# Transposes of the mixture tile loop and of the last stage moved from TensorE to VectorE's 32x32 blocks

## What is computed

```python
x = attention(q, k, v)                    # (1536, 512)
e_idx, gate_w = argmax and softmax weight of x @ w_gate + bias
for e in range(8):                        # one expert per token
    h = np.maximum(x[mask] @ w1[e], 0.0)  # 512 -> 1024
    out[mask] = gate_w[mask, None] * (h @ w2[e])
h = np.maximum(out @ w_in, 0.0)           # 512 -> 2048
return h * h @ w_out                      # 2048 -> 512
```

## Time and profile before

| | before |
|---|---|
| median of three runs | 523.38 us |
| profiled execution, its own time | 523.15 us |
| its span (first to last instruction) | 521.5 us |
| TensorE busy | 510.0 us, 98% |
| VectorE busy | 225.3 us, 43% |
| ScalarE busy | 187.6 us, 36% |
| GpSimd busy | 87.3 us, 17% |
| mean granted TensorE clock | 0.995 |

### The profile page before, as it was taken

How to read it: one execution, slowest core, us unless ns; L and a number is a source line. 1 busy time by engine, 2 the same in 40 slices (tenths; PEclk the granted TensorE clock), 3 DMA queues, 4 the chain that set the end, 5 groups by cost and what they waited for, 6 DMA issues and landing times.

```text
span 521.5 us, 9415 instructions
## 1 busy us (share of the span) xinstructions
PE 510.0 (98%) x3115; PEld 411.3 (79%) x3117; DVE 225.3 (43%) x440; ACT 187.6 (36%) x355; POOL 87.3 (17%) x110
## 2 busy tenths in 40 slices
PE   8899999999999999999999999999999999999995
PEld 3587888878888888888788888888888888888884
DVE  3795786975323544237542422442242234222221
ACT  1875675235423555225522212331221233122121
POOL 4433336017600132200000000300000020000002
PEclk9998999999999999999999999999999999999999
DMA  8999757275571555520200000400000020000002
GB/s 280 308 267 336 258 196 260 79 291 137 124 281 40 201 206 216 192 91 29 94 1 1 0 1 0 161 0 0 0 0 0 0 80 0 0 0 0 0 0 80
DMA packets 19018, 54.92 MB, mean 105 GB/s; under 512 B 2848, under 2 KB 3120, under 8 KB 18480
## 3 DMA queue, kind: packets, MB, share of 16 engines
q1 hardware_dynamic: 11200, 27.47, 16.9%
q0 software_dynamic: 5200, 23.62, 12.4%
q10 hardware_dynamic: 2592, 3.49, 1.8%
HBM read 42.51 MB, written 12.07 MB: 105 GB/s over the span
## 4 chain that ended last, share of the span: by engine, by line
PE 91%; DMA 5%; DVE 2%; ACT 1%; issue 1%; POOLq 0%; POOL 0%; ACTq 0%
PE psum L1652 9%; PE psum L1653 9%; PE psum L1651 9%; PE psum L1667 8%; PE psum L1668 8%; PE psum L1669 8%; PE psum L1535 5%; PE psum L1560 5%; PE psum L1558 5%; PE psum L1537 5%; PE psum L1559 5%; PE psum L1536 5%; DMA q_in<-in_q 3%; PE psum L1568 2%; PE psum L1455 2%; PE psum L1370 2%
## 5 line engine op out<-in xcount | busy, mean ns | idle before, releaser
L1325 DVE TENSOR_TENSOR sq<-r_sb 128x512 f32<-128x512 f32 x48 | 33.2, 692 | 141.5 <-ACT r_sb L733 137.4
L733 ACT ACTIVATE r_sb<-psum 128x512 f32<-128x512 f32 x48 | 28.7, 597 | 143.8 <-PE psum L1653 143.8
L1667 PE MATMUL psum<-W,s_hi 128*128 128x512 f32 x192 | 75.9, 395 | 0.1
L1652 PE MATMUL psum<-z_lo,W 128*128 128x512 f32 x192 | 75.8, 395 | 0.0
L1653 PE MATMUL psum<-z_hi,W 128*128 128x512 f32 x192 | 75.8, 395 | 0.0
L1651 PE MATMUL psum<-z_hi,W 128*128 128x512 f32 x192 | 75.7, 394 | 0.0
L1668 PE MATMUL psum<-W,s_hi 128*128 128x512 f32 x192 | 75.5, 393 | 0.0
L1669 PE MATMUL psum<-W,s_lo 128*128 128x512 f32 x192 | 75.4, 393 | 0.0
L892 POOL DMA_INDIRECT out<-o_sb,sorted_m x12 | 11.6, 967 | 293.3 <-DVE o_sb L1341 291.4
L1327 DVE TENSOR_TENSOR s_lo<-sq,s_hi 128x512 fp32r<-128x512 f32 x48 | 33.2, 692 | 33.5 <-ACT s_hi L735 33.5
L735 ACT ACTIVATE s_hi<-sq 128x512 fp32r<-128x512 f32 x48 | 30.3, 632 | 41.8 <-DVE sq L1325 41.8
(11 more groups left out here) (205 smaller groups left out, 733.0 us busy)
## 6 DMA issues: line engine op xcount, KB each, us to landing
raw<-in_w POOLq DMA_DIRECT2D x4, 2048.0 KB, 9.8
raw<-in_w_io POOLq DMA_DIRECT2D x4, 2048.0 KB, 8.0
v_in<-in_v SPq DMA_DIRECT2D x12, 390.0 KB, 13.3
raw<-in_w SPq DMA_DIRECT2D x8, 512.0 KB, 5.4
kT<-in_kT SPq DMA_DIRECT2D x8, 400.0 KB, 8.0
q_in<-in_q SPq DMA_DIRECT2D x12, 256.0 KB, 9.1
X<-in_vT SPq DMA_DIRECT2D x4, 768.0 KB, 12.3
x_in<-xs_d SPq DMA_DIRECT2D x12, 256.0 KB, 2.7
```

The lines of the kernel that those rows point to most:

```text
L1325: dve.tensor_tensor(sq[:, :], r_sb[:, :], r_sb[:, :], ALU.mult).then_inc(sem["sqs"], 1)
L1652: pe.matmul(bank[f % 2][:, :], wh, z_lo[:, k, :], start=False, stop=False)
L1667: pe.matmul(bank[2 + j][:, :], s_hi[f % SBUFS][:, tok], wh, start=(f == 0), stop=False)
```

## The change

Twelve transposes of TensorE in each step of the tile loop, the 16 of the first group and the 32 of the other two go away. In their place:
- **x.** The load of a tile's rows (from tile 4 on) lands by quarters: partition q*32 + a holds four rows' quarter q of the columns. VectorE then transposes all 32x32 blocks with one instruction (`x_turn`) into `x_w`, which is the memory of `x_lo`; reads and writes step four elements. ScalarE and VectorE split it there.
- **h.** After each half's relu, SP spreads it with four DMAs from `h_sb` to `h_q` (SBUF to SBUF, `spread_h`), and VectorE transposes it (`h_turn`) into `h_w`, the memory of `h_lo`. The first half waits until the first half of `layer2(t - 1)` is done, the second half for its end.
- **z.** The rows of each group land by quarters with four DMAs; VectorE transposes with four instructions a group. The gate is not multiplied on the way in; its square is multiplied onto the output instead (the copies at the end of a group take a scale).
- **Order.** On VectorE, the copy of y comes after both halves of `h_lo`; y has two PSUM banks (4 and 7), and the last `layer2` follows `layer2(n_t - 2)` directly. The rows of w1, w2 and w_in are put in the order 4p + k on the host. TensorE's remaining transposes (tiles 0 to 3) read their operand with a step of four elements.

```diff
             def load_x(t, s):
-                sp.dma_start(x_in[s][:, :], xs_d[bass.ds(row, P), :]).then_inc(s_xs[s], 16)
+                    sp.dma_start(x_in[s][:, :], xs_d[bass.ds(row, P), :].rearrange("(a j) (q f) -> q a j f", a=QW, f=P)
+                                 ).then_inc(s_xs[s], 16)
+            def spread_h(t):
+                for h in range(2):
+                    sp.wait_ge(sem["relu"], t * 2 + (h + 1))
+                    for q in range(KD):
+                        sp.dma_start(h_q[h][q * QW:(q + 1) * QW, :], quarter(h_sb[:, h * DM:(h + 1) * DM], q)
+                                     ).then_inc(s_hq[h], 16)
+            def load_z(g, into):
+                for q in range(KD):
+                    sp.dma_start(into[q * QW:(q + 1) * QW, :], quarter(ys_d[g * GT * P:(g + 1) * GT * P, :], q)
+                                 ).then_inc(sem["zin"], 16)
...
             with sp.Fori(0, (TILES - SPEC) // 2) as m:
                 t = m * 2 + SPEC
+                with sp.If(t < n_t):
+                    with sp.If(t + 1 < n_t):
+                        moe_step(t + 1, 0)
+                    spread_h(t)
+                    with sp.If(t + 2 == n_t):
+                        load_parts()
...
# ScalarE
+                if not isinstance(t, int):
+                    with act.If(t == last):
+                        parts_high()
                 for h in range(2):
                     act.wait_ge(sem["ht"], t * 2 + (h + 1))
+                        act.activation(h_hi[:, 4 * h:4 * h + 4, :], h_w[:, 4 * h:4 * h + 4, :], ACT.Copy
+                                       ).then_inc(sem["hh"], 1)
...
# VectorE
+            def x_turn(t, s, lapx):
+                dve.wait_ge(s_xs[s], lapx * 16)
+                dve.wait_ge(sem["l1"], t * 2)
+                dve.transpose(turned(x_w[:, :, :]), blocks(x_in[s][:, :])).then_inc(sem["x_t"], 1)
+
+            def h_turn(t, h, lap):
+                dve.wait_ge(s_hq[h], lap * (KD * 16))
+                dve.wait_ge(sem["l2" if h else "l2m"], t)
+                dve.transpose(turned(h_w[:, 4 * h:4 * h + 4, :]), blocks(h_q[h][:, :])).then_inc(sem["ht"], 1)
+            def loop_step(t, s, lap):
+                with dve.If(t == last):
+                    parts_turn()
+                x_turn(t + 1, s, lap + 1)
+                x_low(t + 1, True)
+                for h in range(2):
+                    h_turn(t, h, lap * 2 - 1 + s)
+                    h_low(t, (h,))
+                dve.wait_ge(s_ys[s], lap * 16 + 16)
+                y_copy(t - 1, y_sb[s], s)
+                with dve.If(t == last):
+                    z_low(0)
+                    out_low(range(PARTS))
+                    y_copy(last, y_last, 1 - s)
+                low_next(t - 1, range(PARTS, PARTS + 2))
+                low_next(t, range(PARTS))
...
+                    dve.wait_ge(sem["zin"], (g + 2) * (KD * 16))
+                    dve.wait_ge(sem["m1"], g * KFF + KFF)
+                    z_turn(z_in, 0)
+                    for k in range(KD):
+                        if k + 1 < KD:
+                            z_turn(z_in, k + 1)
+                        z_low(g + 1, (k,))
...
# TensorE
                 layer1(t, *weights_of(t), between=((KD // 2, lambda: last.extend(weights_of(t - 1))),))
-                x_transpose(t + 1, s, lapx)
-                layer2(t - 1, *last)
-                h_transpose(t)
+                layer2(t - 1, s, *last)
...
-            part_transposes()
-            layer2(n_t - 1, swapped, n_run)
...
-                    if f == KFF - 1:
-                        with pe.If(g < GROUPS - 1):
-                            z_transpose(g + 1, range(2))
```

More of the change, by code:

```diff
@@ L290, in build @@
     cursor["c"] = after_moe
-    z_part = [sb("c", f"z_part{s}", [P, DM], F32) for s in range(2)] + x_in
+    h_q = [sb("c", "h_q0", [P, DM], F32)]
+    z_q = nc.alloc_sbuf_tensor_at("z_q", [P, GT * DM], F32, offset=cursor["c"])
     z_hi = sb("c", "z_hi", [P, KD, GT * P], F32R)
+    z_w = nc.alloc_sbuf_tensor_at("z_w", [P, KD, GT * P], F32, offset=cursor["c"])
     z_lo = sb("c", "z_lo", [P, KD, GT * P], F32R)
+    h_q.append(sb("c", "h_q1", [P, DM], F32))
+    g_sq = sb("c", "g_sq", [P, NB], F32)
     psum = nc.alloc_psum_tensor("psum", [P, 8, 512], F32)
@@ L329, in build @@
         meta metas sorted rows placed slots rout oh tab n_run e0 x0 warm early lsub scat_b scat_c scat_d x2
-        raw0 raw1 zfill scat_a x_t x_h x_l l1 relu ht hh hl l2 y sh sla slbv slbp
-        counts both ylast wo_h wo_v zin scale zt zh zl m1 r sqs s_h s_l mo o_a o_v out ofree den_ok""".split()
+        raw0 raw1 zfill scat_a x_t x_h x_l l1 relu ht hh hl l2 l2m y sh sla slbv slbp
+        counts both ylast wo_h wo_v zin gsq zt zh zl m1 r sqs s_h s_l mo o_a o_v out ofree den_ok""".split()
     sem = {n: nc.alloc_semaphore("s_" + n) for n in names}
@@ L341, in build @@
     s_ys = [nc.alloc_semaphore(f"s_ys{s}") for s in range(2)]
-    s_part = [nc.alloc_semaphore(f"s_part{j}") for j in range(GT)]
+    s_hq = [nc.alloc_semaphore(f"s_hq{h}") for h in range(2)]
     s_wo = [nc.alloc_semaphore(f"s_wor{s}") for s in range(2)]
@@ L1542, in layer1, with layer2 @@
                         do()
-            def layer2(t, slot, run, between=()):
-                halves = isinstance(t, int)
-                pe.wait_ge(sem["hl"], t * 2 + 1 if halves else t * 2 + 2)
-                pe.wait_ge(sem["y"], t + AHEAD)
+            def layer2(t, s, slot, run, between=()):
+                pe.wait_ge(sem["hl"], t * 2 + 1)
+                if not isinstance(t, int) or t > 1 - AHEAD:
+                    pe.wait_ge(sem["y"], t - 1 + AHEAD)
                 for k in range(KF):
@@ L1551, in layer2 @@
                             do()
-                    if halves and k == KF // 2:
+                    if k == KF // 2:
                         pe.wait_ge(sem["hl"], t * 2 + 2)
@@ L1588, in _ @@
             layer1(1, 0, 1)
-            layer2(0, 0, 1, between=((6, lambda: x_transpose(2, 0, 1)),))
+            layer2(0, 0, 0, 1, between=((6, lambda: x_transpose(2, 0, 1)),))
             h_transpose(1)
@@ L1598, in _ @@
             layer1(2, 0, 1, between=((2, load_counts),))
-            layer2(1, 0, 1, between=((6, lambda: x_transpose(3, 1, 1)),))
+            layer2(1, 1, 0, 1, between=((6, lambda: x_transpose(3, 1, 1)),))
             pe.wait_ge(sem["both"], 1)
```

212 lines of the change are left out of this document (100 added, 112 removed).

## The result

The changed kernel takes 571.86 us (median of four, 569.59 to 572.83) where the kernel before takes 523.44 (522.86 to 523.91): a ratio of 1.094, 95% interval 1.0911 to 1.0968. It is 48.4 us slower. The forecast was 534.2 with a range to 552, so the sign was right and the size was outside the range.

The account below looks back on a forecast made before the run. TensorE, busy 98% of the span, was taken as the bound. From 523.15 us, +13.4 by the end of the tile loop, +1.5 in the last stage and -3.8 for later groups' transposes gave 534.2; forecast 528 to 541, range 513 to 552.

Parts of the forecast that it names:

- What TensorE loses: Whole kernel: TensorE's removed transposes of x, h and z take away 19.5 us, giving 503.6 if nothing waited.
- The ring and its order: Tile loop: relu, spread, turns, y copy and store follow one another without TensorE, back to relu in 9.85 us.
- The recurrence: Tile loop: stepped relu starts and layer1 ends from tile 3; TensorE waits in nearly every step, most 5 us.
- The lap: Tile loop, one tile's relu to the next: 9.85 us, 14.95 with a weight split, against TensorE's 10.99.
- turn, high, low, twice: Tile loop, both halves of h: transpose 0.69, high part 0.59, low part 0.60, twice, 3.76 us.
- y copy to the next relu: Tile loop, end of a lap: y copy 0.69, store issue 0.45, two ScalarE table checks 1.16 us.
- The slow-turn rival: VectorE's turns, mainly in the tile loop, take 1.22 us each instead of 0.69: 546.7 us; chance 0.25.
- Splits: ScalarE in five of nine laps: splitting four weight parts adds 5.1 us, a lap of 14.95.
- Loads: Tile loop, spreads of tiles 4, 5, 7 and 9: a weight load alongside adds 2.8 us to each lap.
- The last tile: End of the tile loop: last layer2 starts at R (its relu's start) + 6.5 and ends 13.4 us later than before.
- The ring fits: Tile loop: laps of 9.2 us, 14.3 with a split, end the loop 3.1 earlier: 517.7 us; chance 0.12.
- Spreads cost more, or the clock falls: Tile loop: spreads beside loads take over 5 us more, or waits lower TensorE's clock: 555 or more; chance 0.10.

Follow-up runs that it names:

- e9_flat2: Changed kernel with h's turns alone read and written without a step, y stores plain, y's rows left in another order: 568.2 us.
- e14_sum: Changed kernel with y store behind next relus, second half's spreads issued by ScalarE, h's turns without a step, weight loads cut to a few columns: 544.9 us.
- e4_hz: Changed kernel with x transposed by TensorE again, h and z still by VectorE: 572.2 us, ratio 1.0987 to the kernel before.
- e11_warm: Changed kernel with 16 added matmuls ahead of each layer 1 of the loop and 56 ahead of the last layer 2: 572.0 us.

## Why the prediction was wrong in size

**What TensorE loses: right.** The last stage gave 3.1 us (predicted 3.84 - 1.5 = 2.3). The turns of z fit at the groups' ends: TensorE goes from down to up without a gap while VectorE turns.

```profile
386.51 0.39 PE L1716 MATMUL psum<-W,s_lo 128*128 128x512 f32 x1
386.74 0.39 PE L1698 MATMUL psum<-z_hi,W 128*128 128x512 f32 x1
```

The strided transposes of tiles 0 to 3 cost nothing that shows, the gate nothing.

**The ring and its order: right.** TensorE waits for x_lo ahead of layer 1 and 9.0 us for h_lo ahead of the last layer 2; relu waits for nothing of TensorE. The recurrence had every lap bound by the ring, and so it was. What failed is the size of the ring's terms.

**The lap, the step that failed: 9.85 us for 13.13, 3.28 too short**, which over nine laps is 29.5 of the 38.6 us by which the sum (11.1 for 49.7) missed. Term by term from the plain lap:
- relu to first issue 0.62 (predicted 0.56);
- issues and landing 164.10 - 159.98 = 4.12 (1.23 + 2.0): +0.89. The three distances between the four issues are 0.64 and not 0.41, which makes 0.69 of it; the earlier trace rows had issues of another shape;
- turn, high, low, twice: 169.15 - 164.10 = 5.05 (3.76): +1.29. The turns are 0.86 of it, taken at 0.69 for 1.12. The rest is handoff, which a sum of durations leaves out: turn start to high start is 1.15 where the turn lasts 1.11, and high to low 0.66 twice, low to turn 0.80;
- y copy to the next relu 172.49 - 169.15 = 3.34 (0.69 + 0.45 + 1.16 = 2.30): +1.04. Of this 2.42 lies between the store's issue and relu.

**The slow-turn rival was true and still too small.** It had 1.22 us and 546.7. Its price was nearly right, but the other three terms were off as well. And taking the price away did not give it back: e9_flat2 gained 3.6 us, not clear of noise, and not 2 x 0.53 a lap, since beside the first turn stood the issue distance of 2.6. On the 16-byte lines the trace agrees with the note in the Trainium skill, SBUF — State Buffer (section "Door 1: the DMA port swizzle"): every element on a new line took 1.04 to 1.07 us for 0.68, and a copy 0.61 for 0.42. The rate of one element per cycle and lane in the Trainium skill, Vector Engine (DVE) Microarchitecture Reference, section 3.8, is compatible with the 0.68 without a step only.

**The other terms of the laps.** Splits: 4.04 for 5.1, five times, 5.3 too much. Loads: 18.8 for 11.2, 7.6 too little, and one of the four laps was the wrong one. First lap: 19.95 against 17.17 for another with a split, 2.8, not in the text at all; the spread of tile 3 was issued at 120.46 and its first half turned at 127.97, 7.5 us later for 4.12, beside GpSimd's twelve indirect transfers of the sort table (115.2 to 131.6 us); no run takes these away, so they are a likely cause and not a shown one. In the other kernels with h in the ring the first lap is 20.0 to 26.0 us. Together 29.5 - 5.3 + 7.6 + 2.8 = 34.6, against 159.85 - 125.4 = 34.5 measured.

**The last tile: 5.1 too short** (17.1 for 12.0). The text let the four z turns hold up ScalarE by 0.7. They hold up VectorE: it waits 2.73 for their landing, turns to 283.8, then turns x (of no use any more) and comes to h at 286.09, 6.4 after relu for 4.7 in a plain lap. Layer 2 starts at 289.22, R + 9.5 for R + 6.5, and takes 7.6 us for 5.5 at the lower clock:

```profile
289.22 0.79 PE L1624 MATMUL psum<-W,h_hi 128*128 x1 [9.01 <-DVE h_lo L1063]
289.81 0.63 PE L1625 MATMUL psum<-W,h_hi 128*128 x1
...
296.83 0.39 PE L1698 MATMUL psum<-z_hi,W 128*128 128x512 f32 x1
```

With 34.5 + 5.1 - 0.8 (last stage) - 0.15 (tile 3's relu) the 11.1 of the prediction come to 49.7, the span's difference.

**The rivals.** "The ring fits" needed laps of 9.2, 14.3 with a split, and 12 us behind the last relu. e14_sum comes near in the laps (10.6 to 11.0, 14.4 to 16.0), but not in the first (22.1) nor in the end (26.6). "Spreads cost more, or the clock falls" (555 or more) named two things that both came: 5.2 us more for a spread beside a load (7.4 for 2.2), and the lower clock in six places, of which 2.1 us at the last tile are on the path. Yet neither is the larger part, which is the plain lap. What was missed in the range: it took the bounds one at a time, the worst as a rival of 0.10, where nearly all unknown durations were short in the same direction (only the split's 5.1 was long).

What stays open: what made the first lap long; how the 2.42 us between the store's issue and relu divide (waits, table reads and branches show no record), and what the clock's fall costs if TensorE is kept busy up to the end of each wait.

## What to carry over

An engine that is busy 98% can be made to wait by work taken from it, if the work goes into a loop of other engines whose lap it did not set before. Before such a move, cost the lap from start to start of neighbouring instructions, not from their durations, and write down each engine's order inside it: here the store ahead of the relu was worth 15 us, taking the step out of h's turns 3.6, not clear of noise. Move first what is known a step ahead (x, z: 1.2% faster together than the kernel before) and leave with the busy engine what has to come back within the step (with h too: 9% slower).

## What the runs showed of the hardware

- A VectorE instruction with two SBUF inputs beside GpSimd work. x_lo read PSUM and SBUF before, now SBUF twice; beside GpSimd's split it took 4.28 us for 0.69:

```profile
141.54 4.28 DVE L1070 TENSOR_TENSOR x_lo<-x_w,x_hi 128x512 fp32r<-128x512 f32 x1 [0.70 <-ACT x_hi L631]
...
140.62 4.65 POOL L876 TENSOR_TENSOR W<-raw,W 128x1024 f32 x2
```

  The Trainium skill, SBUF — State Buffer, section "Who interferes with whom", has this case (two SBUF inputs against a GpSimd instruction that reads SBUF, the later one blocked); the trace agrees in this meeting, where x_lo ended at 145.8 and GpSimd's two instructions at 145.3. In two later laps (213.17 and 252.61) it cost 0.34 only. In e4_hz, where x_lo reads PSUM, it took 0.69 at most and the whole time did not change.
- A DMA issue on SP of 128 partitions x 512 bytes into 32 partitions took 0.60 us (0.55 to 0.80, 80 of them), 0.65 from one to the next; a store of 128 rows of 2 KB on ScalarE 0.35, and 1.05 with the same rows in another order in DRAM.
- From the start of a half's last issue to its landing 2.2 us (161.9 to 164.10) without a load beside it, 7.4 (194.8 to 202.21) beside a load of 2 MB issued at 192.84. In the laps from tiles 4, 7 and 9, and from tile 10 in e4_hz, the half that waited was turned 8.5 to 12.0 us after the load's issue, whichever the kernel, and the loads themselves take 8.8 to 9.3 us (medians) to land: the half came in about with the load, wherever in the lap that was. In the lap from tile 11 it was 13.9 to 14.9, which no run explains.
- In the changed kernel TensorE's lower clock level came back after waits of 6 to 9 us, each time for 8 to 13 matmuls at 0.427 us in place of 0.229, and not after waits of 1.9 to 2.5. In e11_warm, with matmuls ahead of the waits, it came back after 3.15 to 6.2 us, and not after 1.9 and 3.0.
